# First chunk's preparation in a delta-rule attention kernel: inner identities on GpSimd, Gram rounds in four pairs of PSUM banks, square root ahead of the betas

## The reference

```python
# B, H, S, D = 4, 8, 768, 48; float32
k_n = k / (norm(k, axis=-1) + 1e-06)
for t in range(S):
    y[:, :, t] = einsum('bhd,bhde->bhe', q[:, :, t], state)
    v_old = einsum('bhde,bhd->bhe', state, kt)
    state = state + bt * einsum('bhd,bhe->bhde', kt, vt - v_old)
x = transpose(y)                                # (B, S, H * D)
x = mix_1(x, U, V, w_ch1, w_ch2)                # low-rank token mix, MLP
return mix_2(x, w_ch1, w_ch2)                   # real part of a 2-D FFT, layer norm, MLP
```

## Time and profile before

| What | us |
|---|---|
| time, median of 3 runs (1141.83 to 1143.81) | 1141.85 |
| the profiled execution: its own time | 1141.97 |
| its span, first to last instruction | 1140.2 |
| PE busy | 1078.5 (95%) |
| DVE busy | 553.1 (49%) |
| ACT busy | 400.1 (35%) |
| POOL busy | 167.3 (15%) |

### The profile page before, as it was taken

The page is one execution under the profiler, slowest core; times in us unless marked ns, Lnnn a source line. Parts: engine busy times, 40 slices in busy tenths (PEclk is TensorE's granted clock), DMA queues, the critical chain, the costliest instruction groups (busy, mean ns, idle before and its releaser), DMA issues.

```text
span 1140.2 us, 23939 instructions
## 1 busy us (share of the span) xinstructions
PE 1078.5 (95%) x10258; PEld 1025.4 (90%) x10258; DVE 553.1 (49%) x1094; ACT 400.1 (35%) x759; POOL 167.3 (15%) x213
## 2 busy tenths in 40 slices
PE   2699999999999858999999999999999999999998
PEld 1589889888988848999999999999999999999998
DVE  5677777777777315342232234265334434424222
ACT  1566767666666313231111112123212211211211
POOL 1244444444443200000000000000000000000000
PEclk9999999999999767999999999999999999999999
DMA  5112111122222143311002000022010010000001
GB/s 118 34 30 49 43 45 39 40 47 49 48 50 80 64 115 98 125 42 42 1 1 70 1 1 1 1 67 73 1 43 21 1 35 8 22 21 22 21 22 42
DMA packets 86544, 46.50 MB, mean 41 GB/s; under 512 B 53492, under 2 KB 84776, under 8 KB 86440
## 3 DMA queue, kind: packets, MB, share of 16 engines
q1 hardware_dynamic: 86440, 44.98, 14.1%
HBM read 35.53 MB, written 11.85 MB: 42 GB/s over the span
## 4 chain that ended last, share of the span: by engine, by line
PE 62%; DVE 1%; DMA 1%; SPq 0%; ACT 0%; issue 0%; DVEq 0%
PE dn L1376 9%; PE up L1378 9%; PE up L1376 9%; PE dn L1378 9%; PE up L1377 9%; PE dn L1377 9%; PE sd L1376 2%; PE sd L1377 2%; PE sd L1378 2%; PE sd L1433 1%; PE sd L1420 1%; PE sd L1426 0%; DMA stage<-moe_w_ch 0%; DMA stage<-moe_V 0%; DVE work L1292 0%; PE sd L1445 0%
## 5 line engine op out<-in xcount | busy, mean ns | idle before, releaser
L1280 DVE SCALAR_TENSOR_TENSOR hid_l<-up,hid_h 128x384 fp32r<-128x384 f32 x192 | 107.1, 558 | 378.6 <-ACT hid_h L1227 378.5
L1227 ACT ACTIVATE hid_h<-up 128x384 fp32r<-128x384 f32 x192 | 94.3, 491 | 505.3 <-PE up L1378 505.3
L1376 PE MATMUL dn<-w2h,hid_h 128*128 128x384 f32 x576 | 198.7, 345 | 0.4
L1376 PE MATMUL up<-act_h,w1h 128*128 128x384 f32 x576 | 194.6, 338 | 1.2 <-DVE act_l L1296 1.2
L1378 PE MATMUL up<-act_h,w1l 128*128 128x384 f32 x576 | 195.2, 339 | 0.0
L1377 PE MATMUL up<-act_l,w1h 128*128 128x384 f32 x576 | 194.4, 338 | 0.0
L1377 PE MATMUL dn<-w2l,hid_h 128*128 128x384 f32 x576 | 193.9, 337 | 0.0
L1378 PE MATMUL dn<-w2h,hid_l 128*128 128x384 f32 x576 | 193.7, 336 | 0.0
L1376 PEld LDWEIGHTS up<-act_h,w1h 128*128 128x128 f32 x576 | 109.0, 189 | 2.0 <-DVE act_l L1296 1.6
L388 DVE CAST_PREDICATED zi<-merge_mask,zb 128x512 f16<-128x512 uint8 x144 | 98.9, 695 | 24.5 <-PE zb L662 23.2
L1376 PEld LDWEIGHTS dn<-w2h,hid_h 128*128 128x128 f32 x576 | 108.2, 188 | 2.2 <-issue 1.6
(11 more groups left out here) (142 smaller groups left out, 1595.4 us busy)
## 6 DMA issues: line engine op xcount, KB each, us to landing
stage<-moe_w_ch SPq DMA_DIRECT2D x24, 384.0 KB, 3.8
kq_t<-q_t SPq DMA_DIRECT2D x24, 256.0 KB, 3.4
k_raw<-k SPq DMA_DIRECT2D x24, 192.0 KB, 3.6
v_in<-v SPq DMA_DIRECT2D x24, 192.0 KB, 3.2
x_rows<-x_sb SPq DMA_DIRECT2D x6, 384.0 KB
work<-x_sb SPq DMA_DIRECT2D x4, 576.0 KB, 3.9
work<-x_mem SPq DMA_DIRECT2D x4, 576.0 KB, 5.1
y_mem<-x_sb SPq DMA_DIRECT2D x12, 192.0 KB, 6.9
```

Source lines behind the costliest of these rows:

```text
L1227: nc.scalar.activation(hid_h[:, f % 2], up_b[f % 2][:, 0:HALF], ACT.Relu).then_inc(s_hh, 1)
L1280: nc.vector.scalar_tensor_tensor(hid_l[:, f % 2], up_b[f % 2][:, 0:HALF], 0.0, hid_h[:, f % 2], ALU.max, ALU.subtract).then_inc(s_hl, 1)
L1376: nc.tensor.matmul(bank, ah, bh, start=start, stop=False)
```

## The change

Five things are changed, all for the first pair.

1. The twelve `zi` identities go from DVE to POOL, behind `beta_now` of s = -2. DVE's merges of the first inversion wait for them through the new semaphore `s_zi`.
2. DVE writes the four identities `x1`, `x1_t` and `ident_h` ahead of the loop instead, as soon as the identity is loaded. It then waits for the three masks, ahead of its first `square_sums`.
3. The constant loads have three semaphores in place of one, so PE's transposes of the betas wait for the identity and the betas alone.
4. ACT takes the first square root ahead of the two copies of the betas.
5. The four Gram rounds of pair 0 go to four pairs of banks (`pb`, `zb`, `xb`, `cb`), and PE's waits between them are gone.

```diff
-    INITS = 2 + 2 * (LEVELS + 2)
+    INITS = 6
...
+    def gram_bank(pp, g, j, n):
+        return (pb, zb, xb, cb)[2 * g + j if pp == 0 else 0][n]
...
# SP
-            sp.dma_start(ident[:], cst["c_ident"]).then_inc(s_const, 16)
+            sp.dma_start(ident[:], cst["c_ident"]).then_inc(s_ident, 16)
...
# POOL, normalise(), behind beta_now
+                    if s == -2:
+                        eye = ident[:].unsqueeze(1).to_broadcast([C, H, C])
+                        for lv in range(LEVELS):
+                            for g in range(2):
+                                nc.gpsimd.tensor_copy(zi[:, lv, g], eye).then_inc(s_zi, 1)
...
# DVE, ahead of the loop (before: in one_over_norms of s = -2)
-                dve.wait_ge(s_const, 80)
-                for t in [x1, x1_t] + [zi[:, lv] for lv in range(LEVELS)]:
+            dve.wait_ge(s_ident, 16)
+            for t in (x1, x1_t):
+                for g in range(2):
+                    nc.vector.tensor_copy(t[:, g], eye).then_inc(s_init, 1)
+            nc.vector.tensor_copy(ident_h[:], ident[:]).then_inc(s_init, 1)
+            dve.wait_ge(s_init, INITS)
+            dve.wait_ge(s_const, 48)
...
# DVE, merge(lv, g)
+                    if pi == 0:
+                        dve.wait_ge(s_zi, 2 * lv - 1 + g)
...
# DVE, gram(g, j, n), and PE, gram(g, j)
-                            nr[:, pp % NQ, g, h], pb[n][:, 256 * u:256 * u + 256],
+                            nr[:, pp % NQ, g, h], gram_bank(pp, g, j, n)[:, 256 * u:256 * u + 256],
...
-                    else:
+                    elif pp > 0:
                         pe.wait_ge(s_ge, 8 * pp + 4 * g + 2 * j)
...
# ACT, root(): the two beta copies, that stood ahead of the loop
                     nc.scalar.activation(norms[:, 1], norms[:, 0], ACT.Sqrt).then_inc(s_sqrt, 1)
+                    if s == -2:
+                        betas()
...
# PE
-            pe.wait_ge(s_const, 80)
+            pe.wait_ge(s_ident, 16)
+            pe.wait_ge(s_beta_in, 16)
...
-                    pe.wait_ge(s_ge, 8 * pp + 7 + g)
+                    pe.wait_ge(s_ge, 8 * pp + (7 + g if pp else 4 + 4 * g))
```

More of the change, by code:

```diff
@@ L156, in attention @@
     s_const = sem("s_const")
+    s_ident = sem("s_ident")
+    s_beta_in = sem("s_beta_in")
+    s_zi = sem("s_zi")
     s_init = sem("s_init")
@@ L243, in _ @@
             load_keys(0)
-            sp.dma_start(ident[:], cst["c_ident"]).then_inc(s_const, 16)
-            sp.dma_start(beta_rows[:], beta.rearrange("(a b) h (c p) -> (b h c) a p", a=2, p=C)).then_inc(s_const, 16)
+            sp.dma_start(ident[:], cst["c_ident"]).then_inc(s_ident, 16)
+            sp.dma_start(beta_rows[:], beta.rearrange("(a b) h (c p) -> (b h c) a p", a=2, p=C)).then_inc(s_beta_in, 16)
             sp.dma_start(first_mask[:].rearrange("p a n -> p (a n)"), cst["c_first"].bitcast(U8)).then_inc(s_const, 16)
@@ L368, in _ @@
             nc.vector.memset(state[:], 0.0).then_inc(s_init, 1)
-            def identities():
-                dve.wait_ge(s_const, 80)
-                eye = ident[:].unsqueeze(1).to_broadcast([C, H, C])
-                for t in [x1, x1_t] + [zi[:, lv] for lv in range(LEVELS)]:
[L374 to L377, removed]
+            dve.wait_ge(s_ident, 16)
+            eye = ident[:].unsqueeze(1).to_broadcast([C, H, C])
+            for t in (x1, x1_t):
[4 more added lines that the diff above has]
+            dve.wait_ge(s_const, 48)
             def body(s, par, it):
@@ L481, in one_over_norms @@
                     nc.vector.reciprocal(norms[:, 1], norms[:, 1]).then_inc(s_rn, 1)
-                    if s == -2:
-                        identities()
                 merge(1, 1)
@@ L524, in _, with betas @@
         def _(act):
[L525 to L529, removed]
+            def betas():
+                for a in range(2):
+                    act.wait_ge(s_beta_ps, a + 1)
+                    nc.scalar.copy(
+                        beta_t[:].rearrange("p (c b h) -> p b h c", b=B, h=H)[:, 2 * a:2 * a + 2],
+                        pb[a][:, 0:96].rearrange("p (b h c) -> p b h c", b=2, h=H)).then_inc(s_beta, 1)
             def body(s, par, it):
@@ L776, in gram @@
                             pair = kq_t[DP * n:DP * n + DP, pp % NQ, g, 2 * j + u]
-                            last = nc.tensor.matmul(pb[n][:, 256 * u:256 * u + 256], pair[:, 0],
+                            last = nc.tensor.matmul(gram_bank(pp, g, j, n)[:, 256 * u:256 * u + 256], pair[:, 0],
                                                     pair.rearrange("p a t -> p (a t)"), start=True, stop=True)
```

## The result

The changed kernel takes 1130.96 us (median of 4 runs, 1130.53 to 1132.01), the kernel before 1141.84. The ratio is 0.9904, 95% interval 0.9889 to 0.9919. The profiled execution took 1130.91, its span is 1129.1. The forecast was 1130.3, with 1129.0 to 1133.0 as range.

The account below looks back on a forecast made before the run. PE, busy 289.55 of 295 us in the steady steps, bounds the kernel, so only an earlier end of the ramp helps: 4.98 + 6.42 + 0.3 = 11.7 us, 1141.97 - 11.7 = 1130.3 us, range 1129.0 to 1133.0.

Parts of the forecast that it names:

- Norms: Keys' norms in the ramp: sum of squares later, at 8.5, yet square root 0.38 us and `kn`'s end 0.70 us earlier.
- G: End of DVE's last Gram instruction in the ramp, releasing the first inversion: 23.03 instead of 34.73 us.
- Start of the rounds: First Gram round: PE starts at 14.52, DVE reads at 16.63 instead of 21.61, a gain of 4.98 us.
- Rounds: Four Gram rounds of pair 0: 1.68 us apart instead of 3.82, PE limiting slightly, a gain of 6.42 us.
- the 0.3 us of the faster level: PE reaches 2.4 GHz within the unbroken Gram rounds, so DVE limits at 1.58 us per round: 0.3 us gained.
- Clock: PE in the ramp rises from 1.2 to 2.4 GHz: 0.3 us gained, plus 0 to 0.1 in the first inversion.
- clock case: PE at the high or the low clock level in the ramp: 1130.2 to 1130.6 us, chance 0.60 together.
- POOL: Twelve casts on POOL at 1.04 us each, done at 24.4; `keep_t(1)` ends just in time, at no cost.
- The upper bound of 1.11: Dearest plain-copy estimate per POOL cast, 1.11 us; it would cost 0.7 us, with 0.6 of slack behind.
- `first(0)`: DVE instruction beside POOL's casts: no loss expected; by the skill's exclusion rule, up to 1.0 us less gain.
- After the ramp: Steady steps: PE busy 289.55 of 295 us, so all later work begins earlier by whatever the ramp gives up.
- the forecast 11.7: Total gain in the ramp, 4.98 + 6.42 + 0.3 us, taken off the whole time.

Follow-up runs that it names:

- e3_betas_first: Changed kernel with ACT's two beta copies again ahead of the loop and the first square root; 1130.6 us.
- e5_five_late: Changed kernel with DVE's five remaining identity copies (`x1`, `x1_t`, `ident_h`) behind the reciprocal again; 1130.1 us.
- e1_one_pair: Changed kernel with the four Gram rounds of pair 0 back on one pair of banks; 1137.15 us.
- e8_hold: Kernel of e4_filler with more useless PE transposes (8, 4, 6, 6) between the first parts of the first inversion; 1129.15 us.
- e9_all: Kernel of e5_five_late with the four `zi` casts of the last two levels on ACT, plus the fillers of e8_hold; 1128.28 us.
- e10_all_warm: Kernel of e9_all with 14 more useless PE transposes between the betas' and the keys' transposes; 1126.94 us.
- after_again: The changed kernel run once more, unaltered, as reference of the last group; 1131.05 us.
- e4_filler: Changed kernel with useless PE transposes, 32 behind the first turning of N and 16 behind the second; 1130.74 us.
- e6_two_on_act: Changed kernel with the two `zi` casts of the last level on ACT, behind the copies of the keys; 1130.64 us.
- e7_late_hold: Kernel of e5_five_late with the fillers of e8_hold; 1129.85 us.

## Why the prediction was right

- *Norms*: the sum of squares at 8.57 (8.5 forecast), `kn` at 10.34 and 1.47 long (10.29, 1.47). The clash of casts and POOL came as told. Right in size, but e3_betas_first shows that the root's new place alone had no part in it, and e5_five_late that with the twelve on POOL the five casts' new place costs 2.3 to 2.4 us at G.
- *Start of the rounds*: PE at 14.57, DVE at 16.74 (14.52 and 16.63).
- *Rounds*: DVE's four groups start at 16.74 and 21.64 at the ends, 1.63 apart, between the 1.58 and 1.68 of the text. e1_one_pair gives 6.58 for the banks alone, where 6.42 and at most 0.3 more stood.
- *G*: 23.29 for 23.03. The clock rose only with the fourth round, so the 0.3 us of the faster level did not come.
- *Clock*: the step that failed. I had the higher level stay, with 0 to 0.1 us from it; it fell again, and the second pair's preparation lost 1.6 us. Neither clock case of the text had a loss. The time from `beta_now` of pair 1 to the last `kb` settles it, over all fourteen profiled executions. Where the granted clock is 1.00 in the pair's preparation it is 313.04 (before), 313.12 (e1_one_pair), 313.13 (e3_betas_first, whose clock was up again by 33 us) and 313.14 (e8_hold, e9_all, e10_all_warm); where it is at 0.50 in part of it, 313.96 (after_again) to 315.12 (e4_filler), and 314.65 in the changed kernel. e8_hold, in which PE is kept busy, shows the cause as well. The loss is not a fixed one: after_again, the same kernel, lost 0.9 us where the first execution lost 1.6. The other half of what I quoted from the Trainium skill ("TensorE: Matmul & The Clock Gate", Part 1, What's actually happening), that idling drops the level, I did not price. The rows at 21 to 27 us agree with it.
- *POOL*: casts of 1.037 us each (1.04 forecast), and PE's second-level `z_part` at 29.34 did not wait for POOL. Right, and e5_five_late shows how near the edge it was. The upper bound of 1.11 came from the mean of 2278 ns in the earlier trace rows, which mixes copies of 2.10 and 2.78 us; the 2.10 lies on the line of 0.84 ns per column.
- *`first(0)`*: I counted no block. It took 1.13 us, the longest of all pairs, and 0.72 in e6_two_on_act with POOL idle. The line over all pairs (duration ns min/median/max):

```profile
L464 DVE COPY_PREDICATED x<-first_mask,n_h x24: 731/771/1132, 23.2 to 344.9; 128x512 f16<-128x512 uint8 x24
```

`first(0)` began at 23.21, with 0.55 us of POOL's last cast still to run by its record, and took 0.4 us more than in e6. The rule of the Trainium skill ("SBUF — State Buffer", Who interferes with whom) was right in kind. It lay in slack. And I misread the row of 0.78 in the earlier trace rows as no block. The same instruction for g = 0 took 0.73 in the kernel before, with POOL idle (timeline of the kernel before):

```profile
34.65 0.73 DVE L451 COPY_PREDICATED x<-first_mask,n_h 128x512 f16<-128x512 uint8 x1
```

POOL's copy had only 0.21 us of its record left at 35.84, and the stretch was 0.05. In both meetings the stretch is about 0.15 us less than what was left of POOL's record, so that row did not speak against a block.

- *After the ramp*: the shift does pass through the steady steps unchanged, but the seam was 1.2 us shorter. This was in no term. Sum by the terms as measured: 11.44 - 1.61 + 1.22. That the total came within 0.7 us of the forecast 11.7 is partly luck: the clock's loss and the shorter seam are two errors of opposite sign, and the seam is not shown to follow from the change (142.40 in after_again). With the seam of the kernel before, this execution would have taken 1132.1, still inside the range.

What stays open: why the seam takes 140.4 to 141.1 us in some profiled executions and 142.0 to 142.4 in others, the same kernel (changed kernel 140.81, after_again 142.40) among them. TensorE's granted clock changes between 0.50 and 1.00 several times there, so its timing is the likely cause, but no run shows that. No run takes back edit 3 by itself or edits 3 and 4 together. Also open is why the low stretch ends at 38 us in the changed kernel, at 35 in after_again and at 31 in e3_betas_first.

## What to carry to other kernels

In a ramp, price each engine's queue by what stands behind it: twelve casts on POOL were free only because they ended at 23.76, 0.65 us ahead of the first copy behind them, and an improvement upstream made them the limit at once. Giving a latency chain more PSUM banks pays when two engines take turns on one pair (6.6 us here), and moving the twelve casts off DVE, the engine that reads the banks, then pays little (1.9). A faster ramp changes where TensorE idles, and the clock that follows from it took back 0.9 and 1.6 us of 11.4 in two executions of the same kernel; the granted clock by windows of 2 us, and landmarks of one quiet engine in both traces, show where.

## What the runs showed of the hardware

- Fillers of 32 and 16 transposes in TensorE's gaps held the clock at 2.4 GHz to 31 us, another 24 held it to 45 in three of four kernels (not in e7_late_hold, where PE stood 1.33 us for POOL), while 14 float32 transposes at 5.54 to 8.73 did not raise it by 9.67.
- DVE casts and POOL casts of 128x1024 hold each other up (e5_five_late): two DVE casts took 2.13 us instead of 1.28, an `ident_h` copy 1.05 instead of 0.21, and POOL's twelve 13.76 instead of 11.87. DVE's Gram instructions, with one input in PSUM, took 474 to 485 ns beside POOL's casts, as without.
- The granted clock reads 1.00 from the start of every trace, though a Gram round takes 2.08 us there, its length at 1.2 GHz, against 1.04 later. Until that reading has changed once, the durations of matmuls tell the level, and not the reading.
